# One VectorE add over the whole state tile, and a ScalarE scaling of each head's own block

## The reference, cut to what matters

```python
def _attn_ref(q, k, v, alpha):              # B, H, S, D = 2, 8, 768, 48
    state = np.zeros((B, H, D, D))
    for t in range(S):
        state = alpha[:, :, t, :, None] * state + np.einsum('bhd,bhe->bhde', k[:, :, t], v[:, :, t])
        y[:, :, t] = np.einsum('bhd,bhde->bhe', q[:, :, t], state)
```

## Time and profile before

| | |
|---|---|
| time of three runs, median | 484.32 us (484.18 to 486.46) |
| profiled execution's own time | 481.48 us |
| its span | 479.6 us |
| TensorE busy | 432.9 us (90%) |
| VectorE busy | 263.3 us (55%) |
| ScalarE busy | 219.5 us (46%) |
| attention stage | 0 to about 96 us of the span |

### The profile page before, as it was taken

One profiled execution on the slowest core, in us unless ns is written; L12 is line 12 of the kernel. 1 busy time (PEld: TensorE's weight loads), 2 busy tenths in 40 slices (PEclk: granted clock), 3 DMA queues, 4 the chain that ended last, 5 costly groups with the idle time before them and its releaser, 6 DMA issues.

```text
span 479.6 us, 7514 instructions
## 1 busy us (share of the span) xinstructions
PE 432.9 (90%) x2938; PEld 425.7 (89%) x2938; DVE 263.3 (55%) x444; ACT 219.5 (46%) x408; POOL 33.0 (7%) x44
## 2 busy tenths in 40 slices
PE   0899999729999999999981899999999999999996
PEld 0799989619999999999970799999999999999996
DVE  8999999725665666566545343424342334323331
ACT  1254764205556656656645344334442544343332
POOL 4000004700000000000004300200000000000000
PEclk9999999958999999999995699999999999999999
DMA  7789946843667667667774300100000100010001
GB/s 171 204 254 270 277 152 225 296 173 96 210 196 240 209 210 262 207 189 229 217 200 136 91 1 0 51 25 26 1 0 1 50 2 0 1 49 1 0 1 49
DMA packets 38097, 59.65 MB, mean 124 GB/s; under 512 B 2864, under 2 KB 28080, under 8 KB 38064
## 3 DMA queue, kind: packets, MB, share of 16 engines
q1 hardware_dynamic: 36528, 54.48, 37.2%
q0 software_dynamic: 1536, 4.72, 3.0%
HBM read 46.41 MB, written 12.78 MB: 123 GB/s over the span
## 4 chain that ended last, share of the span: by engine, by line
PE 87%; DVE 6%; DMA 4%; issue 2%; ACT 1%; POOL 0%; POOLq 0%; DVEq 0%; ACTq 0%
PE bank L1017 12%; PE bank L1018 12%; PE bank L1019 12%; PE bank L1029 12%; PE bank L1031 12%; PE bank L1030 12%; PE bank L915 4%; PE bank L874 2%; PE bank L893 2%; PE bank L904 2%; PE bank L1004 2%; PE bank L933 1%; DMA slots_y<-arena 1%; DVE bwd L654 1%; DMA slots_x<-x_rows,slot 1%
## 5 line engine op out<-in xcount | busy, mean ns | idle before, releaser
L1017 PE MATMUL bank<-xt_hi,w_hi 128*128 128x256 f32 (+1 forms) x384 | 124.0, 323 | 2.8 <-DVE xt_lo L805 2.8
L1018 PE MATMUL bank<-xt_lo,w_hi 128*128 128x256 f32 (+1 forms) x384 | 121.1, 315 | 0.0
L1019 PE MATMUL bank<-xt_hi,w_lo 128*128 128x256 f32 (+1 forms) x384 | 120.7, 314 | 0.0
L1029 PE MATMUL bank<-w_hi,hid_hi 128*128 128x384 f32 x320 | 108.5, 339 | 0.0
L1031 PE MATMUL bank<-w_hi,hid_lo 128*128 128x384 f32 x320 | 108.1, 338 | 0.0
L1030 PE MATMUL bank<-w_lo,hid_hi 128*128 128x384 f32 x320 | 108.1, 338 | 0.0
L730 DVE TENSOR_TENSOR w_lo<-raw,w_hi 128x1536 fp32r<-128x1536 f32 x40 | 70.0, 1759 | 33.0 <-ACT w_hi L541 32.9
L852 DVE SCALAR_TENSOR_TENSOR arena<-arena,bank 128x384 f32<-128x384 f32 x64 | 35.4, 554 | 90.4 <-ACT arena L621 90.4
L1017 PEld LDWEIGHTS bank<-xt_hi,w_hi 128*128 128x128 f32 x384 | 74.2, 193 | 3.6 <-DVE xt_lo L805 3.6
L1018 PEld LDWEIGHTS bank<-xt_lo,w_hi 128*128 128x128 f32 x384 | 74.3, 193 | 0.0
L1019 PEld LDWEIGHTS bank<-xt_hi,w_lo 128*128 128x128 f32 x384 | 74.2, 193 | 0.0
(11 more groups left out here) (97 smaller groups left out, 382.5 us busy)
## 6 DMA issues: line engine op xcount, KB each, us to landing
raw<-w SPq DMA_DIRECT2D x32, 768.0 KB, 5.0
arena<-qk SPq DMA_DIRECT2D x24, 192.0 KB, 3.7
slots_x<-arena SPq DMA_DIRECT2D x8, 384.0 KB, 4.3
arena<-slots_x SPq DMA_DIRECT2D x8, 384.0 KB, 5.3
slots_y<-arena SPq DMA_DIRECT2D x8, 384.0 KB, 5.6
raw<-w_in SPq DMA_DIRECT2D x4, 768.0 KB, 4.7
raw<-w_out SPq DMA_DIRECT2D x4, 768.0 KB, 6.4
arena<-alpha SPq DMA_DIRECT2D x24, 96.0 KB, 2.6
```

Of the source, the lines that this page charges most:

```text
L1017: pe.matmul(bank_, hi, xt_hi[r][:, kc * BR:kc * BR + n], start=(kc == 0), stop=False)
L1018: pe.matmul(bank_, hi, xt_lo[r][:, kc * BR:kc * BR + n], start=False, stop=False)
L1019: last = pe.matmul(bank_, lo, xt_hi[r][:, kc * BR:kc * BR + n], start=False, stop=(kc == KC - 1))
L1029: pe.matmul(bank_, h_hi, hi, start=(f == 0), stop=False)
```

## The change

`update_state` works on all 128 partitions and all 384 columns in one instruction. The blocks that mix two heads, in `state`, now hold the latest update's cross products. They are never read: `scale_state` scales only the two diagonal blocks of each pair into `decayed`, in eight instructions of 64 partitions x 48 columns in place of four of 128 x 96. The other blocks of `decayed` have to stay zero, so both buffers of it are cleared at the start. The clearing of `state` goes.

```diff
                 for p in range(NPAIR):
-                    last = act.activation(decayed[i % 2][:, p * PR:(p + 1) * PR], state[:, p * PR:(p + 1) * PR], ACT.Copy,
-                                          scale=bwd[i % 4][:, p * SEG:p * SEG + 1])
+                    for j in range(2):
+                        a, b = j * HB, (j + 1) * HB
+                        cols = slice(p * PR + j * D, p * PR + (j + 1) * D)
+                        last = act.activation(decayed[i % 2][a:b, cols], state[a:b, cols], ACT.Copy,
+                                              scale=bwd[i % 4][a:b, p * SEG:p * SEG + 1])
                 last.then_inc(state_scaled, 1)
...
-                for j in range(2):
-                    a, b = j * HB, (j + 1) * HB
-                    s3, d3, u3 = (x[a:b, 0:NPAIR * PR].rearrange("p (h c) -> p h c", h=NPAIR)[:, :, j * D:(j + 1) * D]
-                                  for x in (state, decayed[i % 2], update_bank))
-                    if begins(i):
-                        last = dve.tensor_copy(s3, u3)
-                    else:
-                        last = dve.tensor_tensor(s3, d3, u3, ALU.add)
+                if begins(i):
+                    last = dve.tensor_copy(state, update_bank[:, 0:NPAIR * PR])
+                else:
+                    last = dve.tensor_tensor(state, decayed[i % 2], update_bank[:, 0:NPAIR * PR], ALU.add)
                 last.then_inc(state_updated, 1)
...
-            link(dve.memset(state, 0.0))
+            dve.memset(decayed[0], 0.0)
+            link(dve.memset(decayed[1], 0.0))
```

## The result

The kernel became slower: 490.94 us median of six runs (490.29 to 491.84) against 484.56 us for the kernel before, measured beside it (six runs, 484.18 to 487.85). The ratio is 1.0133, 95% interval 1.0104 to 1.0161. The forecast was 484.1 us with a range up to 486.2 us, so it was wrong; a loss of more than 2.4 us had been given a chance of 0.06. The profiled execution of the kernel after took 491.84 us. Of the kernels further down, e6 and e11 have one execution and e16 has two that took over 1.5% longer than their fastest, and the ratios leave these out while the medians do not.

A forecast was written before the change was run, and what follows sets the result against it. TensorE, busy for 90% of the span, was taken as the bound. Memset +0.44 us against VectorE savings of 0.69 us gave a 0.25 us gain, the new ScalarE stall staying hidden: 484.1 us, range 482.6 to 486.2.

The forecast's parts named there:

- Part 1: One more VectorE memset at the start shifts TensorE's whole sequence by 0.44 us; range 0 to 0.45 us.
- Part 2: One VectorE add replaces two: 0.28 us less, mask another 0.11 us; with the memset the tile 6 one-hot moves -0.25 us.
- Part 3: Eight ScalarE scalings replace four: +0.76 us on each of ten tiles, a new TensorE stall of 0.34 us at tile 6.
- the rival's: ScalarE's halves at alternating partitions do not overlap, 0.32 us each: +0.4 us, up to +0.8 us; chance 0.25.
- the split's wait of 1.00 us for its DMA: On ScalarE in the iteration after tile 6's copy, this wait was to hide the scalings' extra 0.76 us.
- The sum: TensorE begins the ranks at 68.91 in place of 69.16, set by the one-hot: a gain of 0.25 us.
- ScalarE becomes the bound: Scalings at alternating partitions do not overlap; tile 6's copy stalls TensorE 1.1 us: 484.7 us, slower; chance 0.25.
- Data time only: VectorE's merged add gains only 0.15 us per iteration; the one-hot moves +0.12 us: 484.4 us; chance 0.20.
- The stage's end is set otherwise: The last scatter's 4.83 us or the transfer order answers small shifts with a microsecond or two either way; chance 0.10.

The follow-up runs named there:

- e6: The kernel before, unedited, run again (second repeat): 485.43 us, ratio 0.9995.
- e11: Kernel after with its eight scalings grouped by start partition and all scatters held until the last slots are known: 494.62 us, ratio 1.0174.
- e16: Kernel before with plain stores to fixed rows in place of the indirect scatters: 478.73 us, ratio 0.9973.
- e10: Kernel before with the merged add and the two memsets, four full scalings, all scatters held until the last slots are known: 492.24 us, ratio 1.0133.
- e9: Kernel before with all scatters held until the last slots are known: 492.60 us, ratio 1.0142.
- e1: Kernel before with the merged add and the memsets of the kernel after, keeping four full scalings: 480.09 us, ratio 0.9917.
- e7: Kernel after with all scatters held on GpSimd until the last slots are known: 495.18 us, ratio 1.0184.
- e13: Kernel after with four full scalings for tiles 10 and 11, eight for the others: 482.18 us, ratio 1.0069.
- e4: The kernel after, unedited, run again: 489.97 us, ratio 1.0112.
- e8: Kernel after with the second expert's weight loads held until the scatters have landed: 496.38 us, ratio 1.0208.
- e15: Kernel after with plain stores to fixed rows in place of the indirect scatters: 480.15 us, ratio 1.0020.
- e18: The kernel after, unedited, run beside e17: 491.41 us, ratio 1.0135.
- e17: The kernel of e13 run again in another group, where increments come late: 483.66 us, ratio 0.9996.
- e14: Kernel after with four full scalings for tiles up to 9, eight for tiles 10 and 11: 479.24 us, ratio 1.0003.
- e5: The kernel before, unedited, run again (first repeat): 486.1 us, ratio 1.0003.

## Why the prediction failed

**Part 1, the memset: right.** 0.41 us where 0.44 was taken; the second front starts at 17.81 where 17.8 was forecast.

**Part 2, the merged add: right in each duration**, 0.55 us with the next scan 0.46 us behind, the mask 0.61 us behind q_dec. With the scatters held it is worth 0.36 us (e10 against e9), near the forecast's 0.25. What was missed is its worth with late increments, 4 us (e1): the prediction called the last adds of the stage worth nothing, since they lay beside TensorE. In e1's profile TensorE waits 1.42 us for x of tile 10 and keeps its full clock, where the repeats of the kernel before wait 4.2 us and fall to half; why the merged add does that is not shown.

**Part 3, the eight scalings: the step that failed.** It failed in four places.

First, the spacing. I took 0.23 us, the value without a change of start partition, and wrote 0.32 us as the rival's, which decided from 0.28 us. It was 0.345 us: each scaling takes 332 ns, and the next starts a hundredth of a microsecond after its end. The row that decided it was already in the prediction: VectorE's halves at partitions 0 and 64 do not overlap. I gave that 0.25 since no row showed ScalarE; no row showed ScalarE with overlap across start partitions either.

Second, the price of that spacing. The rival said +0.4 us, at most 0.8 us; the stall cost 2.0 us (e7 against e9, by their ratios) to 3.3 us (e13). I let only the copy of tile 6 meet TensorE. Three copies met it: in e4, e7, e8, e13, e15 and e18 TensorE waits 0.49, 1.25 and 0.49 us for x of tiles 4, 6 and 7, all within 0.01 us. In the kernel after it waits 0.49 us at 51.82 for x of tile 4, which it had reached without a wait at 50.47 before. That makes VectorE's mask wait for TensorE (0.88 us at 56.83), the scaling starts at 59.19 and not at 58.33, and the copy of x follows 4.36 us behind it where 3.28 us were forecast. So the stall was 1.25 us and not 0.34 us. For tile 7 I had counted on the split's wait of 1.00 us for its DMA to hide the scalings; in e4 and e7 the split waits for nothing and TensorE stands 0.49 us. In the first profile of the kernel after, half a clock behind it cost another 0.8 us in the update alone.

Third, the claim that from 69 us to the end of the stage ScalarE has over 1 us of slack before the copy at 86.13. It held for the execution that I read. That one lay 3 us under the median of the three runs, and I said so only to shift the sum. In other executions of the same kernel (e6) TensorE waits 4.2 us at that place for that same copy. Then the stage's end is not TensorE's own, but a loop: TensorE's late increment, VectorE's add, the scalings, the logits, the copy of x. With the merged add, eight scalings in place of four in the last two tiles made 7.7 us there (e18 against e17), and nothing where no increment was late (e14, 1.0003).

Fourth, the sum has no term for TensorE's clock. I priced a wait of TensorE by its length alone. From x of tile 10 to x of tile 11 the same work took 4.45 us at a granted clock of 1.00 and 7.83 us at 0.50, so each long wait there cost 3.4 us more than itself. The kernel before pays this in both repeats (e5, e6) and did not in the execution that I read.

**The sum by parts.** Measured by ratios where increments are late: merged add -0.83% (e1); eight scalings up to tile 9 +0.79% (e17 against e1: 0.9996 against 0.9917), eight in tiles 10 and 11 +1.39% (1.0135 against 0.9996). Together +1.35%, or 6.5 us. That these add up is no check: the second and third terms are differences to e1 and e17, so the sum is e18's own ratio, and e1 and e17 ran in different groups, so the middle term is uncertain by about 0.4%. The prediction's range was also added up a little too narrow: 483.6 - 1.2 is 482.4 and 485.1 + 1.2 is 486.3, where it says 482.6 and 486.2. 490.94 us lies outside either.

**The rivals.** "ScalarE becomes the bound" was the right mechanism, with nearly the right spacing, the right place for the early stall, and a price too low: at most 0.8 us for what cost 2.0 to 3.3 us there, and nothing for the end of the stage. "Data time only" is refuted by the 0.46 us step. "The stage's end is set otherwise" named the sensitivity of the end, with the scatters as the reason, and a microsecond or two for it. The runs support its first half: the end did answer by several microseconds, and holding the scatters takes that away. But it isn't the transfer's 4.83 us that grew: the last one takes 2.56 us now. The sentence that a loss of 0.5% would need over half a microsecond for each scaling was wrong for the second, third and fourth reason: the scalings took 0.345 us each.

## What to carry to other kernels

Splitting one instruction into pieces at alternating start partitions costs more than their number says: here eight pieces cost 2.75 us, grouped by partition 2.02 us, and four whole ones 1.17 us. Here the work of keeping the blocks apart did better on an idle engine (two GpSimd memsets a tile, 0.9907) than on the one whose copy TensorE waits for (1.0133). A wait of TensorE is to be priced with the clock of the work behind it, which here cost 3.4 us more where the clock fell. And where the profiled execution lies off the median of the timed ones, no slack read from it may be spent before a second profile shows it too.

## What the hardware showed that was not expected

- ScalarE's scalings overlap their neighbours only at the same start partition: 0.34 to 0.35 us from start to start at alternating ones, 0.22 to 0.24 us at equal ones, for 64 x 48 elements.
- Semaphore increments of TensorE are recorded up to 6 us after the end of their matmuls while GpSimd's indirect scatters run, in 11 of 14 profiles (not in the first of the kernel before, nor in e13 and e14). In the four with the scatters held back they are in time. The cause is open.
- The same wait of TensorE, 1.25 us at the same instruction, was followed by a granted clock of 0.50 for 3.4 us in one execution of the kernel after and by none in two others of the same kernel (e4, e18).
- With the clock at half, the end of the stage takes 7.83 us in place of 4.45 us, and the kernel before shows either in different executions.
